# The first four chunks of a linear-attention kernel: one padded load, a new order on four engines, and the first visit one step later

## The reference

```python
for t in range(S):
    state = alpha[:, :, t, :, None] * state + np.einsum('bhd,bhe->bhde', k[:, :, t], v[:, :, t])
    y[:, :, t] = np.einsum('bhd,bhde->bhe', q[:, :, t], state)
# layer 1: h = x @ w_in;  g = h * tanh(softplus(h));  out = g @ w_out
# layer 2: h = x @ w_in;  g = h * cos(h);             out = g @ w_out
```

## Time and profile before

| | us |
|---|---|
| median of 3 runs | 889.14 |
| lowest, highest | 887.23, 889.53 |
| profiled execution, its own time | 889.28 |
| span of the trace (first to last instruction) | 887.5 |
| busy: PE, DVE, ACT, POOL | 876.0, 418.4, 411.1, 372.2 |

### The profile page before, as it was taken

The page is one execution under the profiler, slowest core; times in us unless marked ns, Lnnn a source line. Parts: engine busy times, 40 slices in busy tenths (PEclk is TensorE's granted clock), DMA queues, the critical chain, the costliest instruction groups (busy, mean ns, idle before and its releaser), DMA issues.

```text
span 887.5 us, 16403 instructions
## 1 busy us (share of the span) xinstructions
PE 876.0 (99%) x6686; PEld 727.4 (82%) x6686; DVE 418.4 (47%) x660; ACT 411.1 (46%) x707; POOL 372.2 (42%) x287
## 2 busy tenths in 40 slices
PE   8899999999999999999999999999999999999998
PEld 7688888888888888888888788888888888888886
DVE  8864322233332222230022766666565666666564
ACT  4444332232333233322455756565565656565554
POOL 3788654444345443432355433323232333323232
PEclk9999999999999999999999999999999999999999
DMA  9635321113212111210133200200200200200000
GB/s 223 191 105 150 88 75 39 40 41 87 64 44 75 39 41 40 75 31 1 54 124 108 72 1 1 71 1 1 72 0 1 72 1 0 72 1 1 37 0 36
DMA packets 17163, 48.28 MB, mean 54 GB/s; under 512 B 2752, under 2 KB 2752, under 8 KB 17088
## 3 DMA queue, kind: packets, MB, share of 16 engines
q1 hardware_dynamic: 17088, 47.23, 18.4%
HBM read 37.79 MB, written 9.44 MB: 53 GB/s over the span
## 4 chain that ended last, share of the span: by engine, by line
PE 94%; DVE 3%; issue 1%; ACT 1%; DMA 0%; POOL 0%; ACTq 0%; DVEq 0%; POOLq 0%
PE low L519 44%; PE low L496 33%; PE pair L496 11%; PE top L453 2%; PE top L434 1%; PE top L439 1%; PE pair L387 1%; PE low L413 1%; PE low L370 1%; DVE growth L724 1%; DVE suffix L713 0%; DMA shared<-aqk_in 0%; DVE w_lo L800 0%; DVE probs L746 0%; ACT w_hi L573 0%
## 5 line engine op out<-in xcount | busy, mean ns | idle before, releaser
L922 POOL TENSOR_TENSOR g_lo<-g,g_hi 128x512 fp32r<-128x512 f32 x192 | 260.9, 1359 | 471.2 <-ACT g_hi L612 471.2
L519 PE MATMUL low<-g_hi,w_hi 128*128 128x512 f32 x576 | 224.6, 390 | 0.3 <-DVE x_out L816 0.3
L519 PE MATMUL low<-g_hi,w_lo 128*128 128x512 f32 x576 | 224.1, 389 | 0.0
L612 ACT ACTIVATE g_hi<-g 128x512 fp32r<-128x512 f32 x192 | 120.6, 628 | 117.7 <-PE low L519 116.9
L519 PE MATMUL low<-g_lo,w_hi 128*128 128x512 f32 x576 | 165.7, 389 | 0.0
L519 PEld LDWEIGHTS low<-g_hi,w_hi 128*128 128x128 f32 x576 | 108.1, 188 | 23.8 <-DVE x_out L816 0.7
L519 PEld LDWEIGHTS low<-g_lo,w_hi 128*128 128x128 f32 x576 | 108.1, 188 | 22.6
L519 PEld LDWEIGHTS low<-g_hi,w_lo 128*128 128x128 f32 x576 | 108.1, 188 | 22.4
L496 PE MATMUL low<-x_hi,w_hi 128*128 128x512 f32 x432 | 124.0, 395 | 1.4 <-DVE w_lo L800 1.0
L496 PE MATMUL low<-x_lo,w_hi 128*128 128x512 f32 x432 | 121.6, 390 | 0.0
L496 PE MATMUL low<-x_hi,w_lo 128*128 128x512 f32 x432 | 121.5, 390 | 0.0
(11 more groups left out here) (107 smaller groups left out, 924.3 us busy)
## 6 DMA issues: line engine op xcount, KB each, us to landing
w_raw<-w_in SPq DMA_DIRECT2D x32, 384.0 KB, 3.1
shared<-aqk_in SPq DMA_DIRECT2D x44, 192.0 KB, 3.7
v_sb<-v_in SPq DMA_DIRECT2D x24, 256.0 KB, 4.4
shared<-aqk_in SPq DMA_DIRECT2D x48, 96.8 KB, 3.8
mid<-x_out SPq DMA_DIRECT2D x6, 768.0 KB, 5.3
shared<-mid SPq DMA_DIRECT2D x6, 768.0 KB, 5.8
out<-x_out SPq DMA_DIRECT2D x5, 768.0 KB, 4.1
out<-x_out SPq DMA_DIRECT2D x3, 256.0 KB, 2.4
```

Of the source, the lines that this page charges most:

```text
L519: mm = nc.tensor.matmul(acc[m], wp[:, f, DM + m * P:DM + (m + 1) * P], gp[:, tile % GB, :], start=(f == 0 and n == 0), stop=(f == FT - 1 a ...
L612: nc.scalar.activation(g_hi[:, tile % GB, :], g[:, tile % GB, :], ACT.Copy).then_inc(ghi_ready, 1)
L922: nc.gpsimd.tensor_tensor(g_lo[:, tile % GB, :], g[:, tile % GB, :], g_hi[:, tile % GB, :].bitcast(F32), ALU.subtract).then_inc(glo_ready, 1)
```

## The change

1. **Loads.** The input `aqk_in` now holds the padding, 112 rows for each chunk. `load_a` and `load_qk` issue one DMA of 112 rows instead of two of 48. The fills of the padding by DVE, ACT and POOL, and their semaphores, are gone.
2. **First four chunks.** DVE runs all masks before `keep_x_lo`, then the splits of pieces 1 and 3, and only then the scans of chunk 4, whose keys and queries it now multiplies too. `add_state` on DVE (line 787: first states added to zeros) is gone; ACT copies each update into the state (`start_state`) right after it is made. ACT makes `w_hi` of pieces 0, 1 and 2 earlier. PE's `values` begins with the first half of the masked scores, and its result uses other banks; the rows of the attention output, and with them of `w_in`, are in another order. POOL waits for the queries of chunk 3 before it splits piece 0.
3. **First visit.** Chunk 4's scores move from step 2 to step 3 and its visit from step 3 to step 4. The visit is now like the later ones: ahead of the step's `first_product`. `prepared_at` is as it was, and DVE's scans for chunk 5 now stand where its name falls, in step 3 behind the mask of chunk 4 and ahead of `add_first(4)` in step 4; those for chunk 6 move from step 4 to step 5.

```diff
@@ -42,6 +42,8 @@
 
+    if s in (3, 4):
+        return BATCH if s == 4 else None
     n = s + FT - 3
...
@@ -50,7 +52,7 @@
 
-    return {2: BATCH, 5: BATCH + 1}.get(s)
+    return {3: BATCH, 5: BATCH + 1}.get(s)
 
...
@@ -250,21 +250,12 @@
                     sp.wait_ge(growth_ready, c - 3)
-                for i in (1, 0):
-                    if c == 0 and i == 0:
-                        sp.wait_ge(a_pad, 1)
-                    if 1 <= c < 4 and i == 0:
-                        sp.wait_ge(a_pads, c)
-                    sp.dma_start(a_of(c)[64 * i:64 * i + D, :], aqk_in[c, i, :, 0:AW]).then_inc(a_in_sem[c % 4], 16)
+                sp.dma_start(a_of(c)[0:ROWS, :], aqk_in[c, :, 0:AW]).then_inc(a_in_sem[c % 4], 16)
 
             def load_qk(c):
                 if c >= BATCH:
                     sp.wait_ge(y_done, c - 3 if c < 6 else c - 1)
-                for i in (1, 0):
-                    if c < BATCH and i == 0:
-                        sp.wait_ge(qk_pad, c + 1)
-                    sp.dma_start(qk_of(c)[64 * i:64 * i + D, :],
-                                 aqk_in[c, i, :, AW:AW + QK]).then_inc(qk_in_sem[qk_buffer(c)], 16)
+                sp.dma_start(qk_of(c)[0:ROWS, :], aqk_in[c, :, AW:AW + QK]).then_inc(qk_in_sem[qk_buffer(c)], 16)
 
...
@@ -418,21 +409,16 @@
                 turn = turn_bank(c)
-                pe.wait_ge(probs_ready, 2 * (c + 1))
                 pe.wait_ge(v_in_sem[c % 3], 16 * (c // 3 + 1))
-                if 2 <= c < BATCH:
-                    pe.wait_ge(xhi_ready, c - 1)
-                    pe.wait_ge(xlo_ready, c - 1)
                 if c >= BATCH:
                     pe.wait_ge(xhi_ready, c)
                     pe.wait_ge(xlo_ready, c)
                     pe.wait_ge(probs_zero, 1)
                 for k in range(2):
+                    pe.wait_ge(probs_ready, 2 * (c + 1) if c >= BATCH else 2 * c + k + 1)
                     for n in range(4):
-                        h = 4 * k + n
-                        at = 32 * (h % 2)
                         nc.tensor.matmul(turn[32 * n:32 * n + 32, k * P:(k + 1) * P],
-                                         v_sb[:, c % 3, h, at:at + 32], probs_of(c, h % 2)[:, h // 2, :],
+                                         v_sb[:, c % 3, 2 * n + k, 32 * k:32 * k + 32], probs_of(c, k)[:, n, :],
                                          start=(k == 0), stop=(c < BATCH), skip_group_check=True)
                 for i in range(2):
                     for n in range(4):
@@ -448,15 +434,16 @@
                         t = HALF * half
                         for k in range(KT):
                             for n in range(4):
-                                p = 2 * k + n // 2 if k < 2 else n
-                                cols = slice(64 * (n % 2), 64 * (n % 2) + 32) if k < 2 else slice(32, 64)
+                                cols = slice(64 * k, 64 * k + 32) if k < 2 else slice(32, 64)
                                 mm = nc.tensor.matmul(turn[32 * n:32 * n + 32, k * P + t:k * P + t + HALF],
-                                                      ahead[0:ROWS, p, cols], q_of(c)[0:ROWS, p, t:t + HALF],
+                                                      ahead[0:ROWS, n, cols], q_of(c)[0:ROWS, n, t:t + HALF],
                                                       start=False, stop=True, skip_group_check=True)
                 mm.then_inc(y_done, 1)
                 if c < BATCH:
                     to = update_of(c)
                     pe.wait_ge(kdt_ready, BATCH if c in (2, 3) else c + 1)
+                    if c in (1, 3):
+                        pe.wait_ge(sum_ready, 2 * c)
                     for p in range(PAIRS):
...
@@ -469,12 +456,14 @@
                 bank = h_of(s)
-                if s == 2:
-                    pe.wait_ge(g_ready, 1)
-                elif 2 < s <= TILES:
+                if s == 0:
+                    pe.wait_ge(probs_ready, 2 * BATCH)
+                elif s == 1:
+                    pe.wait_ge(xlo_ready, BATCH)
+                elif s in (2, 3):
+                    pe.wait_ge(g_ready, s - 1)
+                elif s <= TILES:
                     pe.wait_ge(g_ready, s)
-                if s == 1:
-                    pe.wait_ge(probs_ready, 2 * BATCH)
                 c = next_scores(values_at(s))
...
@@ -525,7 +514,7 @@
                 c = values_at(s)
-                if c is not None and c > BATCH:
+                if c is not None:
                     if next_scores(c) is not None:
                         turn(next_scores(c))
                     halves_update(c)
@@ -537,9 +526,6 @@
                 if scores_at(s) is not None:
                     turn(scores_at(s))
                     scores(scores_at(s))
-                if c == BATCH:
-                    halves_update(c)
-                    values(c)
                 if alive(s - LAG):
...
@@ -579,6 +565,15 @@
 
+            def start_state(c):
+
+                act.wait_ge(state_zero, 1)
+                act.wait_ge(upd_done, c + 1)
+                for i in range(2):
+                    rows = slice(64 * i, 64 * i + D)
+                    nc.scalar.activation(state[rows, c, :, D * i:D * i + D], update_of(c)[rows, :].rearrange(
+                        "d (p e) -> d p e", p=PAIRS), ACT.Copy).then_inc(sum_ready, 1)
+
             def keep_x_hi(c):
...
@@ -666,17 +661,11 @@
                     keep_keys(scores_at(s))
-                if values_at(s) == BATCH:
-                    keep_x_hi(BATCH)
                 jk = x2_split(s)
                 if jk is not None:
                     split_x2(*jk)
 
             act.preload_act_table_set("mish")
-            act.wait_ge(const_ready, 1)
-            for i in range(1, 4):
-                nc.scalar.activation(a_of(i)[32:64, :].rearrange("p (a t) -> p a t", a=PAIRS),
-                                     ones[32:64, 0:1, None].to_broadcast([32, PAIRS, P + 1]), ACT.Copy).then_inc(a_pads, 1)
             act.wait_ge(const_ready, 2)
...
@@ -689,14 +678,18 @@
             keep_x_hi(0)
+            start_state(0)
             keep_keys(2)
+            split_w(0)
+            split_w(1)
             keep_x_hi(1)
-            split_w(0)
+            start_state(1)
             keep_keys(3)
+            split_w(2)
             keep_x_hi(2)
-            split_w(1)
-            split_w(2)
+            start_state(2)
             keep_x_hi(3)
+            start_state(3)
             split_w(3)
...
@@ -840,18 +825,11 @@
                     take_acc(s // FT - 1)
-                if s == 1:
-                    clear_probs()
-                    for c in range(1, BATCH):
-                        add_state(c)
                 if scores_at(s) is not None:
                     mask(scores_at(s))
                 c = values_at(s)
                 if c is not None:
                     add_first(c)
-                    if c == BATCH:
-                        shrink(c + 1)
-                        grow(c + 1)
                     keep_x_lo(c)
                     if next_scores(c) is not None:
                         mask(next_scores(c))
@@ -861,14 +839,13 @@
                 if piece is not None and lo_owner(piece) == 1:
                     split_w(piece)
                 c = prepared_at(s)
-                if c is not None and c > BATCH + 1:
+                if c is not None:
                     shrink(c)
                     grow(c)
                 jk = x2_split(s)
                 if jk is not None:
                     split_x2(*jk)
 
-            nc.vector.memset(a_of(0)[32:64, :], 1.0).then_inc(a_pad, 1)
             nc.vector.memset(suffix[:, :, AW:AW + 1], 1.0).then_inc(scan_const, 1)
...
@@ -893,17 +869,19 @@
             queries(3)
+            mask(2)
+            mask(3)
             keep_x_lo(0)
-            mask(2)
             keep_x_lo(1)
-            mask(3)
             keep_x_lo(2)
             keep_x_lo(3)
             split_w(1)
+            split_w(3)
             shrink(4)
+            keys(4)
             grow(4)
-            add_state(0)
-            split_w(3)
+            queries(4)
+            clear_probs()
             for s in range(STEPS):
...
@@ -967,14 +946,12 @@
             pool.wait_ge(const_ready, 3)
-            for c in range(BATCH):
-                nc.gpsimd.memset(qk_of(c)[32:64, :], 0.0).then_inc(qk_pad, 1)
-            pool.wait_ge(qk_pad, BATCH)
             keys(2)
             keys(3)
+            pool.wait_ge(qd_ready, BATCH)
             split_w(0)
             split_w(2)
-            prepare(4)
+            decay_state(4)
             for s in range(STEPS):
...
@@ -990,8 +967,10 @@
 
-    def flat(x):
-        return x.reshape(CHUNKS, 2, D, -1)
+    def in_rows(x, pad):
+
+        x = x.reshape(CHUNKS, 2, D, -1)
+        return np.concatenate([x[:, 0], np.full((CHUNKS, 64 - D, x.shape[3]), pad, np.float32), x[:, 1]], axis=1)
 
```

(5 more changed lines are left out.)

34 lines of the change are left out of this document (12 added, 22 removed).

## The result

The changed kernel is slower: 893.99 us, median of 20 runs, against 889.18 us of 20 runs of the kernel before on the same chips. The ratio is 1.0043, 95% interval 1.0028 to 1.0058, so 3.8 us more (2.5 to 5.2); the two medians lie 4.8 us apart. The forecast was 888.6 with a range to 891.6.

What follows compares the result with a forecast made beforehand. PE was taken as the bound, busy 876.0 of 887.5 us, so only early waits could change. Gains of 1.4, 1.0 and 2.0 us less losses of 0.5, 2.8 and 0.5 gave 888.6 against 889.14, range 885.0 to 891.6.

Steps and rivals of the forecast that it cites:

- The start, 1.4 us of gain: Up to the first product: 0.6 us from faster loads, 0.8 from DVE and ACT order; first product at 25.4, not 26.8.
- rival D: Loads do not get faster: start gain 0.8, weights piece 2 late by 1.0 us, `x_hi(2)` behind it; 890.2 us, chance 0.11.
- scores possible: After the first four products: `turn(4)` at 34.1, `scores(4)` possible at 34.7 if `queries(4)` is ready.
- Three of DVE's instructions meet POOL here, each at 0 to 3 us: DVE before `scores(4)`: `queries(4)` ends at 35.2, 0.5 us of PE wait, bounds 0 and 2.6.
- `mid_state`, 2.8 us: PE in `values(4)` waits 2.8 us, bounds 0.9 and 4.7, because `add_first(4)` queues behind chunk 5's scans.
- Clock, 1.7 us: Low granted clock behind PE's wait costs 1.7 us, bounds 0 and 2.2, the same as in the kernel before.
- Chunk 6, 0.5 us: Chunk 6's scans, now behind chunk 5's mask, make PE wait 0.5 us, up to 2.4.
- the forecast of 47.65: Forecast end of `first_product(4)` in the changed kernel, 47.65 against 48.14 before, 0.5 us less.
- The forecast's sum by parts: Gains 1.4 (start), 1.0 and 2.0 (waits); losses 0.5 (queries), 2.8 (`mid_state`), 0.5 (chunk 6); low clock paid in both.
- C: POOL ahead of DVE every time, two passes for each of five DVE instructions up to `add_first(4)`: 892.5 us, chance 0.12.
- A: DVE gets its turn: at most one POOL instruction passes ahead of each of DVE's; 886.9 us, chance 0.20.
- The mark: End of `first_product(4)`, 48.14 before; behind it both kernels were taken to have the same work on PE.

Runs made afterwards that it cites:

- experiment 1: Changed kernel, with POOL starting `decay_state(4)` and the row behind it only once DVE has done `queries(4)`: median 894.34 us, ratio 1.0041 to the kernel before.
- experiment 4: Changed kernel, with POOL's first `g_lo` and `w_lo` each waiting for the end of the POOL instruction before: median 889.21 us, ratio 0.9993 to the kernel before.
- experiment 5: Changed kernel, with `keys(4)` and `queries(4)` back on POOL: median 891.37 us, ratio 1.0030 to the kernel before.
- experiment 2: Kernel of experiment 1, with DVE's two scans of chunk 5 put back behind `add_first(4)`: median 889.47 us, ratio 0.9989 to the kernel before.
- experiment 6: Kernel of experiment 5, with DVE's two scans of chunk 5 put back behind `add_first(4)`: median 889.90 us, ratio 0.9998 to the kernel before.
- experiment 8: Kernel of experiment 4, with DVE's two scans of chunk 5 put back behind `add_first(4)`: median 888.06 us, ratio 0.9969 to the kernel before.
- experiment 10: Kernel before, with only the loads changed to one transfer of 112 rows and no padding fills: median 891.13 us, ratio 1.0009 to the kernel before.
- experiment 11: Kernel before, with only the pauses on POOL of experiment 4: median 888.66 us, ratio 0.9967 to the kernel before.
- experiment 9: Kernel of experiment 8, with ACT doing `x_hi(2)` and `start_state(2)` ahead of `w_hi` of piece 2: median 887.56 us, ratio 0.9960 to the kernel before.
- experiment 7: Changed kernel, chunk 5's scans right behind `queries(4)`, POOL held before `w_lo` of piece 4 until they are done: median 889.95 us, ratio 0.9993 to the kernel before.

## Why the prediction was wrong

*The start, 1.4 us of gain.* Measured 0.27: first product at 26.51 in the timeline (26.58 in the chain), not 25.4. `keys(0)` came at 5.80, not 5.5 (6.08 before). From 3 to 16 us the new loads moved 266 GB/s against 226, far from the 397 I leaned on, and carried 17% more. Piece 2 of the weights landed at 24.07 and `x_hi(2)` stood behind it, and PE waited 0.9 us for `start_state(2)`, which I had at under 0.1. That is rival D, whose own figures (0.8 less 1.0) come to -0.2. In place of the 34.7 for "scores possible" stands 35.38: 0.7 late and not 1.1, since the four first products took 8.41 us in a row where I had 6.64 + 2.04.

*The step that failed: "Three of DVE's instructions meet POOL here, each at 0 to 3 us", from which I took half a microsecond of wait for `queries(4)`, bounds 0 and 2.6.* Measured 7.49. Even by its own words the bound was too low: three instructions at up to 3 us each make 9 us, which would have put `queries(4)` at 41.4, and I wrote "over 36". The 4.12 us scan was read as a price of two passes. It was a number cut short from outside: POOL had stopped by itself at 44.52, waiting for that scan. The bound on a pass is the length of POOL's work that depends on nothing DVE still has to do, and I had written that POOL "then has a backlog of `g_lo` and `w_lo` without a gap" in the same paragraph. In the kernel before POOL's `queries(4)` had to wait for the growth scan, which guarded it. That is the first of three rows of POOL in the timeline of the kernel before; the second is the stop that ended the 4.12 us scan, and the third a `w_lo` that had to wait for a DVE scan:

```profile
32.79 1.19 POOL L936 TENSOR_TENSOR shared<-shared,growth 112x512 f32<-112x512 f32 x1 [1.23 <-DVE growth L724]
...
45.77 1.20 POOL L929 TENSOR_TENSOR shared<-shared,suffix 112x512 f32<-112x512 f32 x1 [1.24 <-DVE suffix L713]
...
51.39 2.76 POOL L914 TENSOR_TENSOR w_lo<-w_raw,w_hi 128x768 fp32r<-128x768 f32 x1
```

Moving `keys(4)` and `queries(4)` to DVE took the guard away. Experiments 1 and 4 show the cause, 5 the guard.

*`mid_state`, 2.8 us.* Absent in the changed kernel (-2.8), because the POOL row was over by then. The mechanism was right: where POOL's row still met these scans the wait was 7.3, 2.2 and 4.9 us (experiments 1, 4 and 5), and putting the scans back removed it (2, 6 and 8).

*Clock, 1.7 us.* The granted clock was 0.50, the lower of its two levels (1.2 of 2.4 GHz), from 42.90 to 48.10: 5.2 x 0.5 = 2.6 us, so 0.9 more, behind a stand of 7.49 us instead of 2.0. The term is not fixed by the stand: behind a wait of 2.0 us it was 1.7 us in the kernel before and nothing in experiments 10 and 11, behind one of 1.6 us nothing in experiment 8 and 1.7 in 9. No run here shows what decides, and it puts 1.7 us of chance into every comparison of two profiles here. *Chunk 6, 0.5 us:* no such wait (-0.5).

Together, against the forecast of 47.65: 0.7 + 7.0 - 2.8 + 0.9 - 0.5 = 5.3, and 52.97 was measured. (The forecast's sum by parts, 4.4 of gains less 3.8 of losses, gives 0.6 and not 0.5; nothing hangs on it.)

*The rivals.* C had the mechanism, "POOL ahead of DVE every time", with two passes for each of five instructions and 892.5; it was one instruction, passed by POOL's whole row, and 0.12 was too little for a case whose size nothing in the trace bounded. A ("one pass") rested on scans that met POOL at the end of its row. *The mark* was sound here (4.83 against 4.68) but not in experiments 2, 6, 7 and 8, where the end kept 1.8 to 5.7 us less than the mark had won; PE's waits for POOL's `keys` (1.6 to 3.3 us), and behind them in 2, 6 and 7 a low clock of 1.7 us each, are what the profiles name: 4.0 of 5.0 us, 5.0 of 5.7, 4.1 of 4.0 and, without the clock, 1.6 of 1.8.

## What to carry to other kernels

Before moving work from GpSimd to VectorE, look for the dependences that make GpSimd pause: a VectorE instruction with two inputs in SBUF may be kept out for as long as GpSimd has work that is ready, so bound it by that backlog and not by one instruction. Where such a backlog stands in the way of urgent VectorE work, let GpSimd wait for its own last result at a few places; here the first such pause, of 80 ns, brought a scan from 10.90 to 3.12 us. On the kernel before the same pauses alone gave 0.3% (experiment 11). A wait that has been seen to end may have ended because the other engine starved in turn: check what released it. And before a difference of 2 us between two profiles is put down to a change, look at the granted clock and at how all executions are spread.

## What the runs showed that I had not expected

- A write-only memset in the row lets nothing in, though POOL reads nothing for 0.11 us; a wait for the engine's own semaphore, 80 ns between two records, does. Going by these records it is not the length of the gap that decides; what does stays open.
- It is not all or nothing without pauses: in the kernel before a `w_lo` took 2.76 us at 51.39 (1.8 alone) while a DVE scan ended, and in experiment 5 the same happened twice. It was not that POOL had to wait for its input: the `w_hi` that this `w_lo` reads was done at 49.51. What decides this stays open; it was not tried.
- With transfers of 112 rows the windows at the start show 264 to 268 GB/s at a DMA share of 0.99 to 1.03, with those of 48 rows 226 (both hold loads of the values too); the 377 to 397 GB/s of the 128-row weights was not reached.
